# A chunked recurrence: ak times v in fp16 parts, the dots in another order, the scan an octet sooner, sums of sizes on ScalarE

## The reference, cut to what matters

```
y[t]  = r[t] @ state
Sa    = state @ a[t]
state = state * w[t] - outer(Sa, b[t]) + outer(v[t], k[t])
```

## Time and profile before

| | |
|---|---|
| time, median of 3 | 2124.35 us (2122.78 to 2124.71) |
| the profiled execution | 2122.89 us, span 2120.9 us |
| TensorE busy | 2100.6 us, 99% |
| VectorE busy | 1347.1 us, 64% |
| ScalarE busy | 818.9 us, 39% |
| GpSimd busy | 471.2 us, 22% |
| first x_b, last x_b | 19.20 us, 398.06 us |
| first product of the second layer | 413.72 us |

### The profile page before, as it was taken

The page is one execution under the profiler, slowest core; times in us unless marked ns, Lnnn a source line. Parts: engine busy times, 40 slices in busy tenths (PEclk is TensorE's granted clock), DMA queues, the critical chain, the costliest instruction groups (busy, mean ns, idle before and its releaser), DMA issues.

```text
span 2120.9 us, 36086 instructions
## 1 busy us (share of the span) xinstructions
PE 2100.6 (99%) x14714; PEld 1896.8 (89%) x14714; DVE 1347.1 (64%) x2459; ACT 818.9 (39%) x1464; POOL 471.2 (22%) x424
## 2 busy tenths in 40 slices
PE   8999999899999999999999999999999999999999
PEld 7899998788989988999998999998998998999998
DVE  7888888743656555555555555555555566665665
ACT  4444444332233433333334333333343343433333
POOL 7655555211431201111111112111111010010100
PEclk9999999999999999999999999999999999999999
DMA  7444444311010000000000000000000001011001
GB/s 110 78 73 67 67 71 70 91 53 48 21 48 1 28 28 1 28 28 1 28 28 1 28 16 13 28 1 28 28 1 28 28 1 28 1 28 28 1 26 50
DMA packets 193785, 70.53 MB, mean 33 GB/s; under 512 B 153424, under 2 KB 189776, under 8 KB 193616
## 3 DMA queue, kind: packets, MB, share of 16 engines
q1 hardware_dynamic: 193616, 68.19, 14.6%
HBM read 60.31 MB, written 7.86 MB: 32 GB/s over the span
## 4 chain that ended last, share of the span: by engine, by line
PE 96%; ACT 2%; DVE 2%; issue 0%; POOL 0%; DMA 0%; SPq 0%; DVEq 0%; ACTq 0%
PE up L1481 19%; PE up L1440 13%; PE yps L1538 9%; PE yps L1539 9%; PE yps L1540 9%; PE up L1488 7%; PE yps L1457 4%; PE yps L1455 4%; PE yps L1456 4%; PE yps L1174 3%; PE up L1189 2%; PE misc L1220 2%; PE up L1136 2%; PE up L1197 1%; PE misc L1213 1%; PE up L1174 1%
## 5 line engine op out<-in xcount | busy, mean ns | idle before, releaser
L2015 DVE SCALAR_TENSOR_TENSOR tok<-yps,prob,tok 128x320 f32<-128x320 f32 x672 | 343.0, 546 | 134.7 <-PE yps L1540 134.6
L1538 PE MATMUL yps<-w2h,hh 128*128 128x320 f32 x1344 | 415.0, 309 | 0.5 <-DVE hl L1998 0.4
L1539 PE MATMUL yps<-w2l,hh 128*128 128x320 f32 x1344 | 415.0, 309 | 0.0
L1540 PE MATMUL yps<-w2h,hl 128*128 128x320 f32 x1344 | 415.0, 309 | 0.0
L915 ACT ACTIVATE up<-up 128x512 f32<-128x512 f32 x252 | 146.7, 582 | 396.7 <-PE up L1481 395.0
L1538 PEld LDWEIGHTS yps<-w2h,hh 128*128 128x128 f32 x1344 | 252.3, 188 | 22.2 <-DVE hl L1998 1.4
L1539 PEld LDWEIGHTS yps<-w2l,hh 128*128 128x128 f32 x1344 | 252.3, 188 | 10.5
L1540 PEld LDWEIGHTS yps<-w2h,hl 128*128 128x128 f32 x1344 | 252.4, 188 | 0.0
L718 POOL TENSOR_TENSOR w1l<-w1l_raw,w1h 128x768 fp32r<-128x768 f32 x68 | 103.3, 1518 | 606.5 <-ACT w1h L824 606.5
L1998 DVE SCALAR_TENSOR_TENSOR hl<-up,hh 128x512 fp32r<-128x512 f32 x168 | 115.6, 688 | 161.0 <-ACT hh L927 161.0
L1998 DVE SCALAR_TENSOR_TENSOR hl<-hl_raw,hh 128x512 fp32r<-128x512 f32 x168 | 117.0, 696 | 147.2 <-ACT hh L927 147.2
(11 more groups left out here) (251 smaller groups left out, 4232.5 us busy)
## 6 DMA issues: line engine op xcount, KB each, us to landing
w2l_raw<-in_moe_w SPq DMA_DIRECT2D x16, 640.0 KB, 5.7
w1l_raw<-in_moe_w SPq DMA_DIRECT2D x32, 256.0 KB, 3.1
xr_raw<-x_dram SPq DMA_DIRECT2D x12, 512.0 KB, 4.1
w1l_raw<-in_moe_w SPq DMA_DIRECT2D x32, 128.0 KB, 3.7
wp<-in_w SPq DMA_DIRECT2D x24, 160.0 KB, 3.2
rp<-in_r SPq DMA_DIRECT2D x24, 160.0 KB, 3.1
vp<-in_v SPq DMA_DIRECT2D x48, 80.0 KB, 3.2
raw<-in_a SPq DMA_DIRECT2D x24, 160.0 KB, 3.7
```

The costliest lines, as they stand in the source:

```text
L1538: nc.tensor.matmul(o, hh[:, tile, c], wh, start=first, stop=False)
L1539: nc.tensor.matmul(o, hh[:, tile, c], wl, start=False, stop=False)
L1540: ins = nc.tensor.matmul(o, hl[:, tile, c], wh, start=False, stop=last)
L2015: nc.vector.scalar_tensor_tensor(out=acc, in0=yps[:, s, 0:DM], scalar=prob_of(blk * NSUB + s, e), in1=acc, op0=ALU.mult, op1=ALU.add).then ...
```

## The change

AK is divided by V_SCALE (128) by the mask, v is multiplied by it; both are split into fp16 parts, and AK times v becomes hi.hi + hi.lo + lo.hi (24 products of 40 columns). ScalarE makes v_s (fp32), v_hi and ak_hi, GpSimd v_lo and ak_lo. The tiles vp, bt and kt lose their empty slots, v is loaded in one DMA and not two. The dots a.k come before a.b, the transposes of k before those of b, and k is scaled before b. The dots r.v move from the end of the octet before to between the second and the third round, y_by_head with kt from there to behind the dots a.k. w is transposed and scanned two octets ahead. The sizes of N and w are summed on ScalarE by an absolute value with an accumulated output, halves of N apart, and sizes_bounded comes later in the last octet.

```diff
-                pe.wait_ge(c_akm, 2 * o + 2)
-                by_head(pz, ak_t, vp[:, buf], first=empty, last=True).then_inc(c_x, 1)
+                pe.wait_ge(c_vh, o + 1)
+                pe.wait_ge(c_akh, 2 * o + 2)
+                by_part(pz, ak_hi, v_hi, first=empty)
+                pe.wait_ge(c_vl, o + 1)
+                by_part(pz, ak_hi, v_lo)
+                pe.wait_ge(c_akl, 2 * o + 2)
+                by_part(pz, ak_lo, v_hi, last=True).then_inc(c_x, 1)
...
-                rough_by_head(pu, [n_hi], x_b).then_inc(c_zj, 1)
+                rough(pu, x_b).then_inc(c_zj, 1)
+                if 0 <= o - 1 < UPDATES:
+                    state_by_rows(tj, o - 1)
                 if following:
-                    w_by_tokens(tj, *following)
-                    slots_by_channels(tj, vp[:, 1 - buf])
+                    by_channels(tj, rp[:, 1 - buf])
...
+                by_part(pz, n_hi, z_b, first=True)
                 pe.wait_ge(c_nlo, 2 * o + 2)
-                rough_by_head(pz, [n_hi, n_lo], z_b).then_inc(c_zj, 1)
-                if 0 <= o - 1 < UPDATES:
-                    state_by_rows(tj, o - 1)
+                by_part(pz, n_lo, z_b, last=True).then_inc(c_zj, 1)
+                value_query(tj, buf)
+                pe.wait_ge(c_za, o * NEWS + 2)
+                rough(pz, zz).then_inc(c_zj, 1)
...
+                if after:
+                    pe.wait_ge(c_ta, a_done)
+                    w_by_channels(*after)
                 pe.wait_ge(c_ta, sa_done)
                 pe.wait_ge(c_zd, o + 1)
                 dots(both(rs_banks), sa_t, r_t[:, buf], c_rs)
                 if following:
-                    b_by_channels(tj, *following)
-                    b_done = tj.now()
+                    k_by_channels(tj, *following)
+                    k_done = tj.now()
                     if not empty or bb + 1 == B:
                         pe.wait_ge(c_ta, a_done)
                         a_state(*following)
-                    k_by_channels(tj, *following)
-                    k_done = tj.now()
+                    b_by_channels(tj, *following)
+                    b_done = tj.now()
+                    pe.wait_ge(c_rsm, 2 * o + 2)
+                    pe.wait_ge(c_ta, k_done)
+                    dots(both(ak_banks), k_t, a_t, c_ak)
+                pe.wait_ge(c_rvm, 2 * o + 2)
+                y_by_head(kt[:, buf], rv_t, first=empty)
                 if not last:
                     pe.wait_ge(c_s, o + 1)
                 if following:
+                    if after:
+                        pe.wait_ge(c_scan, o + 3)
                     pe.wait_ge(c_ta, b_done)
                     dots(both(n_banks), b_t, a_t, c_n)
-                    dots(both(ak_banks), k_t, a_t, c_ak)
-                    value_query(tj, 1 - buf)
```

More of the change, by code:

```diff
@@ L226, in build @@
         ak_t = chunk_sb("ak_t", [P, PAIRS, 2, P])
+        ak_hi = chunk_sb("ak_hi", [P, PAIRS, 2, P], F16)
+        ak_lo = chunk_sb("ak_lo", [P, PAIRS, 2, P], F16)
+        v_s = chunk_sb("v_s", [P, H, D])
+        v_hi = chunk_sb("v_hi", [P, H, D], F16)
+        v_lo = chunk_sb("v_lo", [P, H, D], F16)
+        unread_n = chunk_sb("unread_n", [P, 2, PAIRS, P], F16)
+        unread_w = chunk_sb("unread_w", [P, 2, DM], F16)
         rv_t = chunk_sb("rv_t", [P, PAIRS, 2, P])
@@ L1282, in octet @@
                     y_state(buf, bb)
-                else:
-                    pe.wait_ge(c_rvm, 2 * o + 2)
-                    y_by_head(kt[:, buf], rv_t, first=empty)
-                pe.wait_ge(c_za, o * NEWS + 2)
-                rough_by_head(pz, [n_hi], zz).then_inc(c_zj, 1)
-                if not last:
-                    for p in range(PAIRS):
-                        nc.tensor.matmul(of_pair(pu, p)[0:PR, 0:PR], heads_of(kt[:, buf], p), heads_of(vp[:, buf], p),
-                                         start=(p == 0), stop=False, skip_group_check=True)
-                if o in LATE:
-                    pe.wait_ge(c_rvm, 2 * o + 2)
-                    y_by_head(kt[:, buf], rv_t)
                 pe.wait_ge(c_again, o + 1)
-                rough_by_head(yps[:, 2, :], [n_hi], z_b).then_inc(c_zj, 1)
+                rough(yps[:, 2, :], z_b).then_inc(c_zj, 1)
                 if following:
-                    by_channels(tj, rp[:, 1 - buf])
+                    by_channels(tj, vp[:, 1 - buf])
                     a_by_channels(tj, *following)
@@ L1341, in chunk @@
                 for bb in range(B):
[L1342 removed]
+                    octet(tj, g, bb, at_octet(g * B + bb + 1), at_octet(g * B + bb + 2), last)
             pe.wait_ge(s_sel, 1)
@@ L1715, in octet @@
                 z_new = zf[:, :, 0:D]
-                if following:
-                    wait(dve, c_ya, o - (o in LATE))
-                    scan(*following)
-                else:
-                    sizes_bounded(dd)
+                if not following:
                     solved(slice(0, OCT - 1), 2, dd)
@@ L1791, in chunk @@
                 for bb in range(B):
-                    octet(dd, g, bb, (g, bb + 1) if bb + 1 < B else None if last else (g + 1, 0), last)
+                    octet(dd, g, bb, at_octet(g * B + bb + 1), at_octet(g * B + bb + 2), last)
             dd = Count(0)
```

252 lines of the change are left out of this document (123 added, 129 removed).

## The result

The changed kernel takes 2135.68 us (median of 4 runs, 2135.05 to 2138.05) against 2124.53 for the kernel before in the same session (2122.78 to 2124.79): 11.15 us more, ratio 1.0056 with a 95% interval of 1.0039 to 1.0074. I had forecast 2121.0, range 2110 to 2130. It is slower, and outside the range.

The account below looks back on a forecast made before the run. TensorE, busy 99%, was taken as the bound. Terms 0.7 + 2.9 + 0.8 - 5.0 - 0.1 - 2.3 + 0.3 - 1.7 = -4.4, +1.1 for accumulating copies = -3.3 us; forecast 2121.0 us, range 2110 to 2130.

Parts of the forecast that it names:

- The first octets and the clock: Octets 0 to 4: GpSimd's weight splits delay n_lo, TensorE waits 1.8, 1.8, 2.9 us; +2.9 us, plus +0.8 for the clock.
- the clock once, +0.8: The new 2.9 us wait in octet 4 could lower TensorE's clock once, 0 to 1.7 us, taken as +0.8.
- the walk: Adding up the four queues instruction by instruction, x_b to x_b, with 0.06 us handovers; it gave 16.56 for the old octet.
- Octet 0: First of the five opening intervals, forecast to change by -0.3 us against the old order.
- Ak times v, the steady octet: Fp16 sets take 0.60 for 1.79 us; of 1.10 saved 0.36 is left, 16.20 per octet; -5.0 us over 14 intervals.
- the accumulating copy: ScalarE's absolute-value sums of sizes: 0.25 us extra for each of four, +1.1 us in all, nothing in the steady octet.
- rival C: GpSimd becomes the bound in the octets as its instructions get 0.1 to 0.2 us dearer: 2125 to 2131 us; chance 0.23.
- rival D: The absolute value makes ScalarE reload its table, over 5 us per octet, some +130 us; chance 0.02.
- The start: Before the first x_b: GpSimd clears mt and mb, then makes v_lo and ak_lo, so x_b starts at 19.9; +0.7 us.
- The end: Octet 23: wait for z_b falls from 3.3 to 1.2 us, -2.3; kt.rv later, +0.3; clock stays up, -1.7.
- -1.7 for a clock that stays up: Octet 23: with the z_b wait so short TensorE's clock was expected to stay up, worth -1.7 us.
- Octets 19 to 22: ak_lo waited for 1.2 to 1.3 us, -0.1 in sum; load of w up to 0.5 each in octets 20 and 21.

Follow-up runs that it names:

- bridge: Changed kernel plus TensorE matmuls on constants in five long waits (octets 0, 2 to 4, 23), every wait kept: 2127.75 us, 1.001 of the kernel before.
- all_fills: Changed kernel with mt/mb cleared early, weight splits before ak_lo, first x_lo after the last correction, loads ahead, and constant matmuls in TensorE's waits: 2119.76 us, 0.9982.
- no_sums: Changed kernel with the sums of sizes of N and w left out of ScalarE's queue altogether: 2137.44 us in one run.
- early_fill: Changed kernel with GpSimd clearing mt and mb before its first wait: 2137.78 us, 1.0064 of the kernel before.
- loads: Changed kernel with SP issuing the next octets' w and raw loads, and the output three octets back, before its wait for the rounds: 2141.1 us in one run.
- mask_dve: all_fills with octet 23's mask of rv_t moved from GpSimd to VectorE and all x_lo after the verdict: 2118.17 us, 0.9971 of the kernel before.
- narrow_before: Kernel before with only ak times v narrowed from 128 to 40 columns, still fp32: 2125.27 us, ratio 1.0006.
- split_gap: Changed kernel with GpSimd's splits of the first expert's weights moved from after ak_lo to between v_lo and ak_lo: 2124.66 us, 1.0004 of the kernel before.
- tail: Changed kernel with VectorE's first x_lo of octet 23 made after the last correction of z: 2137.77 us, 1.0057 of the kernel before.

## Why the prediction was wrong, step by step

- *The first octets and the clock*: this is the step that failed. The waits for n_lo were right (1.75, 1.56, 2.35 for 1.8, 1.8, 2.9). The next term, "the clock once, +0.8", was not. I had one row of a fallen clock, after a wait of 2.5 us, and gave only the longest wait a chance of it. The clock fell in octets 0, 2, 3 and 4, to means of 0.78, 0.91, 0.83 and 0.92, and bridge puts its price at 4.7 us in octets 2 to 4 and 2.4 in octet 0: 7.1 for the 0.8. For the five intervals I had 85.0 before the clock; they took 93.68. With the clock held up (bridge) octets 2 to 4 take 17.81, 17.95 and 18.99, near the 17.5, 17.4 and 18.6 of the walk.
- *Octet 0*: 15.5 said, at a full clock; 18.55 measured. The wait of 1.86 us for ak_lo stands ahead of its x_b, and the clock falls inside that wait and stays at 0.50 until about 28.5 us. With constants in the waits the octet takes 16.0 (all_fills).
- *Ak times v, the steady octet*: the sum was right, -4.4 for -5.0 and 16.24 for 16.20, and partly by luck. The three sets take 0.20 each, and ak_lo at 1163 ns and n_lo at 1165 are as in the earlier trace rows. But I had 0.92 us of waits and "about 0.08" that comes back in TensorE's own work, though the two prices named beside it (0.99 against 0.89, two sets) make 0.2. From the start of one group to the next, the mean of 11 octets, the dots r.v take 1.09 us for 0.99 before, a.k 1.09 for 0.89, a.b 1.10 for 1.00, and y_state 1.00 for 0.90: 0.50 more work. The waits are 0.37 for r_t (forecast 0.46), 0.07 for z_b (0.22) and 0.13 at the last ak set and y_state (0.24 with the output): 0.57. The steady part of the saving was eaten by work as much as by waits. Two of the dots, a.k and a.b, in the chain of the changed kernel, with y_by_head between them:

```profile
189.65 1.09 PE yps L1220 x16
190.74 1.02 PE up L1235 x16
191.76 1.09 PE yps L1220 x16
```

- *The rivals*: the accumulating copy has a price that I had bounded, an instruction of its own with means of 0.19 to 0.22 us; no_sums puts all the sums at 0.07 per steady octet. The slower result is what rival C forecast, but not by its way: GpSimd's instructions did not get dearer. For rival D the trace has one table load, as before.
- *The start*: +0.7 said, +1.04 measured. early_fill takes away 0.97.
- *The end*: -3.7 said, +3.07 measured. I counted the instructions that VectorE loses before z_b and never wrote down the rest of octet 23. The first z_b of VectorE starts 2.80 us after x_b for 3.75 before, 0.95 sooner and not some 2 us. The walk also had TensorE wait 3.3 us there in the kernel before, where its trace has 2.51. The verdict's row took 3.6 us instead of 2.6, since it now stands beside n_lo: its second instruction is 1.19 for 0.35. Then comes VectorE's x_lo beside GpSimd's later mask of rv_t, 1.69 us instead of 0.68, ahead of the last correction, for which TensorE waited 2.10 (the verdict's row of the kernel before, then three rows of the changed one):

```profile
400.36 0.35 DVE L1699 TENSOR_TENSOR st_d<-st_d,st_norm 128x184 f32<-128x184 f32 x1
```

```profile
406.91 1.19 DVE L1736 TENSOR_TENSOR st_d<-st_d,st_least 128x184 f32<-128x184 f32 x1
...
414.41 1.69 DVE L1713 TENSOR_TENSOR xl<-xr_raw,xh 128x512 fp32r<-128x512 f32 x1 [0.58 <-ACT xh L864]
...
416.56 0.66 PE L1196 MATMUL up<-ident,zf 128*128 128x128 f32 x4 [2.10 <-DVE zf L1701]
```

With the clock fallen twice in this stretch, -1.7 for a clock that stays up was wrong too. The other order of the end brings 14.16, which is 1.5 under the kernel before, so even then most of the -3.7 isn't there.
- *Octets 19 to 22*: -0.1 said, +0.98 measured. I put the load of w inside the range as "up to 0.5 each"; TensorE waited 1.55 for it once. loads removes that wait.

The terms missed by 0.3 (start), 8.7 less the 0.8 for the clock (octets 0 to 4), 0.6 (steady), 1.1 (octets 19 to 22) and 6.8 (end), less the 1.1 I had allowed for accumulating copies: 15.5 us, which is 12.24 + 3.3. What stays open is why the clock falls in one place and not in another: after waits of about 1 us in octets 1 and 21 of bridge and not in the changed kernel, after z_b's 1.6 us in all_fills and not in mask_dve, and without a long wait in narrow_before.

## What to carry to other kernels

A queue walk that gets the waits right still has to price what TensorE does after each: here waits of 1.6 to 2.4 us, in a kernel 99% busy before, came back nearly doubled in octets 2 to 4 (11.0 us for 5.7, of which 4.7 through the clock). So when the steady loop moves, walk the first and the last passes just as carefully, every engine and queue of them, for there the fillers and the slack differ. Move a filler first (split_gap: 11 us for a few lines), and only then judge the arithmetic. One trace is not enough for a stretch in which the clock falls: the same code of octets 2 to 4 took 59.2 to 62.7 us in the traces of early_fill, the changed kernel, tail and loads.

## What was not expected of the hardware

- After waits of 1.6 to 2.4 us TensorE's granted clock read 0.50 (1.2 GHz) for about 3 us in octet 2 and for 6.6 us in octet 1 of bridge. The fall came 1 to 2 us after the wait had ended in octets 2 and 4 and in octet 1 of bridge, and inside the wait in octets 0 and 3. In narrow_before the clock fell in octets 0, 1 and 3 with no wait over 0.7 us shown.
- GpSimd's PARTITION_ALL_REDUCE started 5.5 to 5.9 us after GpSimd's previous instruction in the ten kernels that had one shortly before; where GpSimd had been idle for over 8 us it started 0.14 us after its releaser.
- A VectorE instruction with both inputs in SBUF took 1.08 us for 128x8 elements beside a GpSimd tensor_tensor, 0.17 alone.
- An activation that also accumulates is followed by an ACTIVATION_READ_ACCUMULATOR on ScalarE, mean 0.19 to 0.22 us. The next instruction starts about 0.09 us after it has started.
- Narrowing the fp32 products from 128 to 40 columns changed neither the mean of an instruction (275 and 277 ns) nor the octet (16.54 us).
